# First units with gate products in pairs and a short warm-up, and MLP pieces through four stages, in a fused attention, MLP and expert kernel

## The chip, the cores and the metric

The kernel runs on one core of a Trainium2 chip, as one program. The metric is the device time of one execution in microseconds (us), the median of several executions. The engines are named as in the profile: PE (TensorE), PEld (its weight loads), DVE (VectorE), ACT (ScalarE), POOL (GpSimd) and SP (SyncE, which here only issues DMAs). A matmul's result stands in PSUM, eight banks of 128 partitions by 512 words; GpSimd is never given a PSUM operand here.

## The reference, cut to what matters

Three layers follow one another over 3072 tokens (4 sequences of 768) with 384 features (8 heads of 48):

```
# 1. linear attention with decay, per batch and head
y[t] = r[t] @ (state + (u * k[t]) outer v[t])
state = w[t][:, None] * state + k[t] outer v[t]
# 2. MLP:            x = (relu(x @ w_in) ** 2) @ w_out          384 -> 2048 -> 384
# 3. experts, top 1 of 8, on tokens with x @ w_skip > 0
out = x + prob * (relu(x @ w1[e]) @ w2[e])                      384 -> 1024 -> 384
```

All inputs and outputs are float32. The kernel takes each large product as three: every operand is split into a rounded high half (ScalarE's copy) and the low half that is left (a subtraction), and hi x hi, hi x lo and lo x hi are summed (`three`, line 565).

## The kernel before, in words

**Chunks and units.** The 768 time steps are cut into 6 chunks of 128 steps. A unit is one chunk of one sequence, four units a chunk, 24 in all. `chunk(i, par, c, cg)` is written out on every engine: its loop over f = 0 to 15 computes the MLP of chunk i, one block of 128 hidden features a turn (`layer1` on TensorE, `relu` on ScalarE, `square` on VectorE, `square_hi` and `square_lo`, and `layer2` two turns later), and between the pieces `side(n, ...)` with n = 2f and 2f+1 puts the attention of the four units of chunk c = i+1, eight steps a unit, and the routing of chunk i-1. Chunks 1 to 4 are a hardware loop; chunk 0 and the last are written out. Before chunk 0 stands a part of its own, the first four units, whose attention nothing of the MLP accompanies. It is there that most of the change lies.

**One unit.** DMAs bring r, k and the decays w with time along the free axis (`load_rk`, `load_decays`), v, and r and k once more with time along the partitions (`load_own`). VectorE takes the running product of the decays (`decays`, L1108) and its reciprocal in two halves (`inverse`, L1119). GpSimd multiplies (`factors`): r by the running product (L1472), then r by k and by u in the "own" rows (L1477, L1479), then k by the inverse (L1481). VectorE sums the own rows by head (`own_term`, L1139), and ScalarE puts those sums on the diagonal of the score tiles, eight copies (`own_diagonal`, L928). TensorE multiplies k by r (`head_scores`, L617), VectorE copies the scores under a mask over the diagonals (`mask_scores`, L1127), TensorE transposes k (`k_transpose`, L626), multiplies scores by v (`attention`, L646 to L662) and k by v (`growth`, L686). ScalarE takes k and the attention's high half out of PSUM (`take_k` L906, `take_xhi` L915), VectorE the low half and the new state (`take_xlo` L1169, `grow_state` L1153). An engine works through its own list in order; semaphores are the only thing that orders engines among themselves.

**Order before chunk 0.** TensorE begins with `keep_busy(8)`: matmuls whose results nobody reads, 8 of 512 columns (L773) and 32 of 128 columns (L777), the second kind on tiles that GpSimd clears. Then, unit by unit: scores, three gate products, from unit 2 on a gate turn, transposes, attention, growth. VectorE does decays and inverses of units 0 and 1 before unit 0's mask, and then in each unit those of the unit two later.

**The gate.** The router's weights are carried through the MLP: w_out times w_gate (with w_skip as further columns) is computed once and appended to w_out. w_out comes transposed in four pieces (n = 0 to 3) through `x2[0]` and `x2[1]`. `gate_product(n, k)` (L697) is one of three matmuls of a piece, 512 columns each, into ACC[0]; ScalarE copies the sum out (`take_gate`, L1008, after `own_diagonal` of the next unit), the next piece's first product waits for that copy, and `gate_turn(n)` (L706) turns it by four transposes. `wo_hi` and `wo_lo` then take the result (L1019, L1353), which `layer2(0, 0)` waits for.

**The MLP's weights.** Eight pieces of 768 KB, w_in and w_out by turns, k = 0 to 7. Each goes through a stage, `stage[k % 2]`: SP loads it when GpSimd has taken the low half of piece k-2 (`load_mlp_piece`, L386), ScalarE copies the high half (`split_hi`, L894), GpSimd subtracts, in three or four parts (`split_lo`, L1499), and counts `w_lo`. Pieces 0 and 1 are split before chunk 0, the high halves of 2 to 7 in chunk 0 at f = 1, 2, 4, 6, 8 and 10. Layer 1 waits for `w_lo` 1, 3, 5, 7 at f = 0, 4, 8, 12 and layer 2 for 2, 4, 6, 8. One queue, SP's, issues all these loads in a written order; an issue that waits holds every one behind it.

## Time and profile before

| | us |
|---|---|
| median of 3 runs | 813.08 (812.76 to 816.14) |
| the profiled execution's own time | 818.62 |
| its span | 817.0 |
| TensorE busy in the span | 775.0 (95%), 5539 matmuls |
| VectorE, ScalarE, GpSimd busy | 455.4, 325.3, 279.8 |
| mean granted clock of TensorE | 0.978 |
| time from span start to the MLP's first matmul | 55.78 |

The busy shares are over the whole span, in which the stages have different limits. The part before the MLP's first matmul is 7% of the span; its limits are seen only in the timelines of the engines. The granted clock is a share of TensorE's full speed: 1.00 is the upper of its two levels, 2.4 GHz, and 0.50 the lower, 1.2 GHz. The starts of instructions are those of the profile; where a line stands for several instructions, its length runs from the first one's start to the last one's end.

### The profile page before, as it was taken

How to read it: one execution, taken by the hardware profiler on the slowest of the kernel's cores; microseconds unless marked ns; L12 is line 12 of the kernel's file. 1: busy time of each engine (PE TensorE's matmuls, PEld its weight loads, DVE VectorE, ACT ScalarE, POOL GpSimd, SP SyncE). 2: the span in 40 equal slices, each digit the busy share in tenths (PEclk: the TensorE clock that was granted, in tenths of full speed). 3: DMA queues.
4: the chain of work that ended last, by engine and by line, in shares of the span. 5: the costliest groups of instructions: out<-in, count | busy, mean ns of one | idle time of the engine just before them, and what ended most of it. 6: DMA issues, size and time to landing. Idle time of an engine off the chain costs nothing.

```text
span 817.0 us, 15673 instructions
## 1 busy us (share of the span) xinstructions
PE 775.0 (95%) x5539; PEld 668.8 (82%) x5539; DVE 455.4 (56%) x733; ACT 325.3 (40%) x629; POOL 279.8 (34%) x280
## 2 busy tenths in 40 slices
PE   7879999999999998999999999999899999999884
PEld 4357788888888887888888898998799999999774
DVE  7757876766676665766586635334422244244841
ACT  1444443433343333433343324343422255255621
POOL 6366662222224220522142310282420025241840
PEclk9889999999999999999999999999899999999988
DMA  8762522422233223322232005344432136445610
GB/s 260 221 185 60 151 63 59 128 59 59 60 97 89 60 59 102 89 59 59 82 105 52 16 25 193 134 148 166 156 126 68 58 126 204 149 136 175 244 36 7
DMA packets 52351, 88.31 MB, mean 108 GB/s; under 512 B 5948, under 2 KB 33832, under 8 KB 52272
## 3 DMA queue, kind: packets, MB, share of 16 engines
q1 hardware_dynamic: 42192, 62.19, 26.6%
q0 software_dynamic: 5504, 16.44, 5.6%
q10 hardware_dynamic: 4576, 8.65, 3.1%
q8 instruction: 46, 0.75, 0.4%
q14 instruction: 33, 0.27, 0.1%
HBM read 72.98 MB, written 16.75 MB: 110 GB/s over the span
## 4 chain that ended last, share of the span: by engine, by line
PE 90%; issue 4%; DVE 3%; ACT 3%; DVEq 0%; POOL 0%; POOLq 0%; ACTq 0%
PE bank L567 26%; PE bank L569 24%; PE bank L568 24%; PE bank L617 3%; PE bank L825 2%; PE bank L662 2%; PE bank L646 2%; PE bank L697 1%; ACT spare L928 1%; PE bank L686 1%; PE bank L626 1%; PE bank L773 1%; PE bank L764 1%; PE bank L651 1%; PE bank L656 1%
## 5 line engine op out<-in xcount | busy, mean ns | idle before, releaser
L567 PE MATMUL bank<-wo_hi,h_hi 128*128 128x394 f32 (+1 forms) x576 | 202.1, 351 | 1.6 <-DVE h_lo L1396 1.5
L569 PE MATMUL bank<-wo_hi,h_lo 128*128 128x394 f32 (+1 forms) x576 | 196.6, 341 | 0.0
L568 PE MATMUL bank<-wo_lo,h_hi 128*128 128x394 f32 (+1 forms) x576 | 196.4, 341 | 0.0
L1282 DVE SCALAR_TENSOR_TENSOR hid<-bank,hid 128x512 f32<-128x512 f32 x96 | 65.1, 678 | 152.0 <-ACT hid L958 152.0
L958 ACT ACTIVATE hid<-bank 128x512 f32<-128x512 f32 x96 | 57.0, 594 | 168.3 <-PE bank L569 161.3
L567 PE MATMUL bank<-xt_hi,wi_hi 128*128 128x512 f32 x288 | 118.7, 412 | 2.2 <-issue 2.2
L1472 POOL TENSOR_TENSOR work<-work 112x512 f32<-112x512 f32 x24 | 28.4, 1185 | 257.5 <-DVE work L1108 248.3
L567 PEld LDWEIGHTS bank<-wo_hi,h_hi 128*128 128x128 f32 x576 | 109.1, 189 | 7.6 <-DVE h_lo L1396 2.2
L569 PE MATMUL bank<-xt_hi,wi_lo 128*128 128x512 f32 x288 | 113.5, 394 | 0.0
L568 PE MATMUL bank<-xt_lo,wi_hi 128*128 128x512 f32 x288 | 113.4, 394 | 0.0
L568 PEld LDWEIGHTS bank<-wo_lo,h_hi 128*128 128x128 f32 x576 | 109.1, 189 | 3.0
L569 PEld LDWEIGHTS bank<-wo_hi,h_lo 128*128 128x128 f32 x576 | 108.9, 189 | 0.0
L967 ACT ACTIVATE h_hi<-hid 128x512 fp32r<-128x512 f32 x96 | 60.6, 631 | 85.6 <-DVE hid L1282 83.8
L1119 DVE RECIPROCAL odds<-work 112x256 f32<-112x256 f32 x48 | 83.2, 1741 | 0.7
L1589 POOL DMA_INDIRECT out<-odds,y_idx x26 | 26.1, 1003 | 153.5 <-issue 142.5
L1288 DVE TENSOR_TENSOR h_lo<-hid,h_hi 128x512 fp32r<-128x512 f32 x96 | 70.5, 734 | 12.5 <-ACT h_hi L967 12.1
L928 ACT ACTIVATE spare<-ident,own_sum 128x128 f32<-128x128 f32 x192 | 58.8, 389 | 38.3 <-DVE own_sum L1139 35.6
L1232 DVE TENSOR_TENSOR xt_lo<-bank,xt_hi 128x384 fp32r<-128x384 f32 x25 | 13.9, 556 | 107.8 <-ACT xt_hi L976 107.8
L567 PE MATMUL bank<-wi_hi,xt_hi 128*128 128x512 f32 x144 | 60.3, 419 | 9.5 <-DVE xt_lo L1232 5.5
L1030 ACT ACTIVATE hid<-bank 128x512 f32<-128x512 f32 x48 | 28.7, 598 | 101.5 <-PE bank L569 98.4
L567 PEld LDWEIGHTS bank<-xt_hi,wi_hi 128*128 128x128 f32 x288 | 54.4, 189 | 16.5 <-issue 6.5
L569 PEld LDWEIGHTS bank<-xt_hi,wi_lo 128*128 128x128 f32 x288 | 54.5, 189 | 12.4
(143 smaller groups left out, 1264.7 us busy)
## 6 DMA issues: line engine op xcount, KB each, us to landing
work<-rkw SPq DMA_DIRECT2D x48, 192.0 KB, 3.6
spare<-rk_rows SPq DMA_DIRECT2D x23, 384.0 KB, 4.3
work<-v_rows SPq DMA_DIRECT2D x25, 192.0 KB, 3.9
work<-sorted_rows SPq DMA_DIRECT2D x24, 193.0 KB
work<-rkw SPq DMA_DIRECT2D x48, 96.0 KB, 3.2
x_cur<-sorted_rows SPq DMA_DIRECT2D x24, 192.0 KB
x<-w POOLq DMA_DIRECT2D x6, 768.0 KB, 6.3
work<-w ACTq DMA_DIRECT2D x6, 768.0 KB, 7.4
```

The source lines that it names most:

```text
L567: pe.matmul(ps, a_hi, b_hi, start=start, stop=False, skip_group_check=True)
L568: pe.matmul(ps, a_hi, b_lo, start=False, stop=False, skip_group_check=True)
L569: return pe.matmul(ps, a_lo, b_hi, start=False, stop=stop, skip_group_check=True)
L928: last = act.activation(scores[:, h % 2, h // 2, :], ident[:, :], ACT.Copy, scale=own_sum[:, b % 2, h:h + 1])
L958: act.activation(hid[:, f % 2, :], HID[f % 2][:, :], ACT.Relu).then_inc(sb_relu, 1)
L967: act.activation(h_hi[:, f % 3, :], hid[:, f % 2, :], ACT.Copy).then_inc(sb_hhi, 1)
L1030: act.activation(hid[:, half, :], banks[2 + half][:, :], ACT.Relu).then_inc(e_relu, 1)
L1119: dve.reciprocal(inv[0:PK, :].rearrange("p (j t) -> p j t", j=PAIRS)[:, two], by_time(cum[b % 2])[0:PK, two, 1:T + 1]).then_inc(inv_done, 1)
L1282: dve.scalar_tensor_tensor(hid[:, f % 2, :], HID[f % 2][:, :], 0.0, hid[:, f % 2, :], ALU.max, ALU.mult).then_inc(sb_sq, 1)
L1288: dve.tensor_tensor(h_lo[:, f % 3, :], hid[:, f % 2, :], h_hi[:, f % 3, :].bitcast(F32), ALU.subtract).then_inc(sb_hlo, 1)
L1472: pool.tensor_tensor(r, r, by_time(cum[n])[0:PK, :, 0:T], ALU.mult).then_inc(r_done, 1)
L1589: pool.indirect_dma_start(out=out, out_offset=bass.IndirectOffsetOnAxis(ap=y_idx[:, n:n + 1], axis=0), in_=y_out[:, n, :], in_offset=None, ...
```

## The change

- **Warm-up.** `keep_busy(3)` in place of 8, and the small matmuls go, with GpSimd's clearing of their tiles. VectorE's clearing of `state` goes to GpSimd, and VectorE waits for it before the first `grow_state`. `const_v` counts one step more, so that the loads into unit 0's tiles can start as soon as their own padding is set.
- **First loads.** Own rows of unit 0 and `u_rows` are issued before r and k. `factors(..., own_first=True)` multiplies the own rows before r in units 0 to 4.
- **VectorE's order.** Unit 0's masks come before the inverses of unit 1; in the last units scan and half of the inverse of unit (1,0) come before `take_xlo(0, 0, 3)`.
- **Gate products.** Two at a time: after unit 0's growth, then before `k_transpose` and after the gate turn of units 1 to 3, into the banks HID[0] and HID[1] by turns. ScalarE's `take_gate` comes ahead of the unit's `take_k`, and `own_diagonal` after `split_hi`. `layer1(0, f)` with f < 2 waits for the copies out of HID.
- **MLP pieces.** Four stages, `stage[0]`, `stage[1]`, `x2[0]`, `x2[1]`: piece k waits for `w_lo` of k-4, pieces 2 and 3 for the gate products that read `x2`. Their places on SP's queue and those of `split_lo` on GpSimd's list change. `take_sums(0)` waits until all pieces are split.
- **Chunk 0.** Its side steps run two places later (`late=2`): none in f = 0, and the last two after the loop.

The diff, cut to its core:

```diff
@@ semaphores and stages
-        w_loaded = [sem(f"w_loaded{n}") for n in range(2)]
+        w_loaded = [sem(f"w_loaded{n}") for n in range(4)]
+        MLP_STAGES = stage[0:2] + [x.rearrange("p b d -> p (b d)")[:, 0:STAGE] for x in x2]
...
-            return (first_piece, second_piece)[k % 2](k % 2, k // 2)
+            return (first_piece, second_piece)[k % 2](k % 4, k // 2)
@@ SP
-                if k >= 2:
-                    sp.wait_ge(w_lo, k - 1)
+                if k >= 4:
+                    sp.wait_ge(w_lo, k - 3)
+                elif k >= 2:
+                    sp.wait_ge(ps_wg, k + 1)
...
             load_decays(0, 0, 1)
-            load_rk(0, 0, 1)
+            load_own(0, 0)
             sp.wait_ge(const_v, 1)
             load_decays(0, 0, 0)
+            sp.dma_start(own_u[:, :], u_rows).then_inc(u_loaded, 16)
+            load_rk(0, 0, 1)
+            sp.wait_ge(const_v, 2)
             load_rk(0, 0, 0)
-            load_own(0, 0)
-            sp.dma_start(own_u[:, :], u_rows).then_inc(u_loaded, 16)
...
             load_transposed(1)
-            load_mlp_piece(0)
             early_decays(3)
             early_rk(2)
+            load_mlp_piece(0)
             load_mlp_piece(1)
...
             load_own(1, 0)
+            load_mlp_piece(2)
             early_v(4)
+            load_mlp_piece(3)
             early_decays(5)
             early_rk(5)
+            load_mlp_piece(4)
+            early_v(5)
+            load_mlp_piece(5)
             load_own(1, 1)
-            early_v(5)
-            load_mlp_piece(2)
-            load_mlp_piece(3)
-            load_mlp_piece(4)
+            load_mlp_piece(6)
             refill(1, 2)
-            load_mlp_piece(5)
-            load_mlp_piece(6)
             load_mlp_piece(7)
@@ PE
+                if isinstance(i, int) and i == 0 and f < 2:
+                    pe.wait_ge(sb_wg, f + 3)
...
-                    if n > 0:
-                        pe.wait_ge(sb_wg, n)
-                last = pe.matmul(ACC[0][0:NG, :], gate_w[:, k, :], transposed_piece(n)[:, k, :],
+                    if n >= 2:
+                        pe.wait_ge(sb_wg, n - 1)
+                last = pe.matmul(HID[n % 2][0:NG, :], gate_w[:, k, :], transposed_piece(n)[:, k, :],
...
+            def gate_products(first):
+                for n in range(first, first + 2):
+                    gate_product(n // KD, n % KD)
...
-            keep_busy(8)
+            keep_busy(3)
             for b in range(B):
                 head_scores(0, b)
-                if b == 0:
-                    pe.wait_ge(const_dma, 16)
-                for k in range(KD):
-                    gate_product(b, k)
-                if b > 1:
-                    gate_turn(b - 2)
+                if b > 0:
+                    gate_products(4 * b - 2)
                 k_transpose(0, b)
                 attention(0, b)
                 growth(0, b)
-            gate_turn(B - 2)
+                if b > 0:
+                    gate_turn(b - 1)
+                if b == 0:
+                    pe.wait_ge(const_dma, 16)
+                if b < B - 1:
+                    gate_products(4 * b)
             gate_turn(B - 1)
-            chunk(0, 0, 1, None)
+            chunk(0, 0, 1, None, 2)
@@ ACT
             for b in range(B):
+                if b > 0:
+                    take_gate(b - 1)
                 take_k(0, b)
                 take_xhi(0, 0, b)
-                own_diagonal((b + 1) // B, (b + 1) % B)
-                take_gate(b)
+                if b == B - 1:
+                    take_gate(b)
+                    act.wait_ge(ps_wg_turned, 4)
+                    act.activation(wo_hi[:, :, DM:], WG_PS, ACT.Copy).then_inc(wg_hi, 1)
                 if b in (1, 2):
                     split_hi(b - 1)
+                own_diagonal((b + 1) // B, (b + 1) % B)
@@ DVE
-            dve.memset(state[:, :, :, :], 0.0)
...
+            decays(0, 0)
+            inverses(0, 0)
+            own_term(0, 0)
+            decays(0, 1)
             mask_scores(0, 0, 0)
             mask_scores(0, 0, 1)
+            inverses(0, 1)
             own_term(0, 1)
+            dve.wait_ge(state_cleared, 1)
+            for b in range(2):
                 take_xlo(0, 0, b)
                 grow_state(0, b)
+                decays(0, b + 2)
+                mask_scores(0, b + 1, 0)
+                mask_scores(0, b + 1, 1)
+                inverses(0, b + 2)
+                own_term(0, b + 2)
+            take_xlo(0, 0, 2)
+            grow_state(0, 2)
+            mask_scores(0, 3, 0)
+            mask_scores(0, 3, 1)
+            decays(1, 0)
+            inverse(1, 0, 0)
+            take_xlo(0, 0, 3)
+            grow_state(0, 3)
+            own_term(1, 0)
+            inverse(1, 0, 1)
@@ POOL
-            pool.memset(h_lo[:, 0, 0:T].bitcast(F32), 0.0)
-            pool.memset(h_hi[:, :, :].bitcast(F32), 0.0).then_inc(h_clear, 1)
+            pool.memset(state[:, :, :, :], 0.0).then_inc(state_cleared, 1)
...
-            for b in range(B):
-                factors(0, b)
+            for b in range(3):
+                factors(0, b, own_first=True)
             split_lo(0)
-            factors(1, 0)
+            factors(0, 3, own_first=True)
             split_lo(1)
+            factors(1, 0, own_first=True)
+            split_lo(2)
             factors(1, 1)
-            for k in (2, 3, 4):
+            for k in (3, 4):
                 split_lo(k)
```

## Rows read from the trace of the kernel before

**Rows 1.** The page: the chain that ended last, by engine.

```profile
PE 775.0 (95%) x5539; PEld 668.8 (82%) x5539; DVE 455.4 (56%) x733; ACT 325.3 (40%) x629; POOL 279.8 (34%) x280
PEclk9889999999999999999999999999899999999988
PE 90%; issue 4%; DVE 3%; ACT 3%; DVEq 0%; POOL 0%; POOLq 0%; ACTq 0%
```

**Rows 2.** Chain that ended last, 0 to 110 us: start us, length us, what.

```profile
5.29 9.57 PE bank L773 x16
...
55.78 0.73 PE bank L567
```

**Rows 3.** TensorE in order of time: start, length, operation, idle time before.

```profile
18.31 1.16 PE L617 MATMUL bank<-work 48*128 48x128 f32 x16
...
27.21 4.43 PE L697 MATMUL bank<-x,gate_w 128*10 128x512 f32 x6 [1.91 <-ACT hid L1008]
...
46.55 2.73 PE L697 MATMUL bank<-x,gate_w 128*10 128x512 f32 x6 [1.91 <-ACT hid L1008]
...
55.19 0.60 PE L706 MATMUL bank<-ident,hid 10*128 10x10 f32 x4 [3.16 <-ACT hid L1008]
...
59.85 1.91 PE L617 MATMUL bank<-work 48*128 48x128 f32 x16
...
75.33 0.40 PE L567 MATMUL bank<-xt_hi,wi_hi 128*128 128x512 f32 x1
...
78.93 1.16 PE L617 MATMUL bank<-work 48*128 48x128 f32 x16 [1.35 <-issue]
```

**Rows 4.** VectorE in order of time, same columns.

```profile
5.26 1.23 DVE L1108 TENSOR_TENSOR_SCAN work<-work,odds 112x516 f32<-112x516 f32 x1
...
11.48 1.81 DVE L1108 TENSOR_TENSOR_SCAN work<-work,odds 112x516 f32<-112x516 f32 x1
...
19.64 1.33 DVE L1127 COPY_PREDICATED spare<-before,bank 128x512 f32<-128x512 int32 x2 [2.94 <-PE bank L617]
...
28.12 3.35 DVE L1119 RECIPROCAL odds<-work 112x256 f32<-112x256 f32 x2
...
40.91 0.49 DVE L1139 TENSOR_REDUCE own_sum<-spare 128x8 f32<-128x384 f32 x1
...
43.63 0.56 DVE L1169 TENSOR_TENSOR xt_lo<-bank,xt_hi 128x384 fp32r<-128x384 f32 x1 [2.23 <-ACT xt_hi L915]
44.11 0.71 DVE L1153 TENSOR_TENSOR spare<-bank,work 48x192 f32<-48x192 f32 x2
...
47.16 1.36 DVE L1127 COPY_PREDICATED spare<-before,bank 128x512 f32<-128x512 int32 x2
```

**Rows 5.** GpSimd in order of time, same columns.

```profile
4.45 1.37 POOL L1534 MEMSET h_hi<- 128x1536 f32 x1
...
8.91 0.99 POOL L1477 TENSOR_TENSOR spare<-spare 128x384 f32<-128x384 f32 x1 [1.09 <-DMA odds<-u_rows]
...
10.94 1.26 POOL L1481 TENSOR_TENSOR work<-work,odds 112x512 f32<-112x512 f32 x1
...
70.68 4.24 POOL L1499 TENSOR_TENSOR wi_lo<-stage,wi_hi 128x512 fp32r<-128x512 f32 x3
```

**Rows 6.** ScalarE in order of time, same columns.

```profile
24.16 2.43 ACT L928 ACTIVATE spare<-ident,own_sum 128x128 f32<-128x128 f32 x8
...
33.27 0.49 ACT L915 ACTIVATE xt_hi<-bank 128x384 fp32r<-128x384 f32 x1 [0.51 <-PE bank L656]
...
146.60 0.25 ACT L985 ACTIVATE logits<-bank 128x10 f32<-128x10 f32 x2 [0.70 <-PE bank L569]
```

**Rows 7.** Stretches of 2 us: PE, PEld, DVE, ACT, POOL busy, clock, DMA.

```profile
28.00:30.00 2.00, 2.00 (x4) 0.38 (x3) 2.00 (x3) 0.00 (x0) 1.92 (x3) 0.50 1.05 385
...
56.00:58.00 2.00, 2.00 (x5) 1.54 (x5) 0.32 (x1) 0.13 (x1) 0.66 (x1) 0.50 0.84 300
```

**Rows 8.** DMA issues over the span: what, KB each, median us to landing.

```profile
x<-w_out_t SPq DMA_DIRECT2D x4, 768.0 KB, 7.1
```

More of the change, by code:

```diff
@@ L746, in side, with chunk @@
                     rows_transpose(0)
-            def chunk(i, par, c, cg):
+            def chunk(i, par, c, cg, late=0):
                 for f in range(NF):
                     layer1(i, par, f)
-                    side(2 * f, c, cg)
+                    side(2 * f - late, c, cg)
                     if f >= 2:
@@ L754, in chunk @@
                     if f < NF - 1:
-                        side(2 * f + 1, c, cg)
+                        side(2 * f + 1 - late, c, cg)
                 layer2(i, NF - 2)
-                side(2 * NF - 1, c, cg)
+                for n in range(2 * NF - 1 - late, 2 * NF):
+                    side(n, c, cg)
                 layer2(i, NF - 1)
@@ L773, in keep_busy @@
                     pe.matmul(HID[1][:, :], before[:, :], start_col[:, 0:512], start=True, stop=True)
-                pe.wait_ge(h_clear, 1)
-                for q in range(4 * n):
-                    cols = slice(q % 4 * T, q % 4 * T + T)
-                    pe.matmul(HID[1][:, 0:T], h_hi[:, q % 3, cols], h_lo[:, 0, 0:T], start=True, stop=True)
-            keep_busy(8)
+            keep_busy(3)
             for b in range(B):
                 head_scores(0, b)
-                if b == 0:
-                    pe.wait_ge(const_dma, 16)
-                for k in range(KD):
-                    gate_product(b, k)
-                if b > 1:
-                    gate_turn(b - 2)
+                if b > 0:
+                    gate_products(4 * b - 2)
                 k_transpose(0, b)
@@ L980, in take_sums @@
                 act.wait_ge(ps_acc, NF * i + NF)
+                if isinstance(i, int) and i == 0:
+                    act.wait_ge(w_lo, MLP_PIECES)
                 if not (isinstance(i, int) and i < 2):
@@ L987, in take_sums, with chunk @@
                     act.activation(x2[par][:, b, 0:DM], ACC[b][:, 0:DM], ACT.Copy).then_inc(x2_act, 1)
-            def chunk(i, par, c, cg, c_last=False):
+            def chunk(i, par, c, cg, c_last=False, late=0):
                 for f in range(NF):
@@ L997, in chunk @@
                     relu(i, f)
-                    side(2 * f, c, cg, par, c_last)
+                    side(2 * f - late, c, cg, par, c_last)
                     square_hi(i, f)
-                    side(2 * f + 1, c, cg, par, c_last)
+                    side(2 * f + 1 - late, c, cg, par, c_last)
+                for n in range(2 * NF - late, 2 * NF):
+                    side(n, c, cg, par, c_last)
                 take_sums(i, par)
@@ L1296, in take_sums @@
             def take_sums(i, par):
+                if isinstance(i, int) and i == 0:
+                    dve.wait_ge(w_lo, MLP_PIECES)
                 if not (isinstance(i, int) and i < 2):
@@ L1301, in take_sums, with chunk @@
                     dve.tensor_copy(x2[par][:, b, 0:DM], ACC[b][:, 0:DM]).then_inc(x2_dve, 1)
-            def chunk(i, par, c, cg, c_last=False):
+            def chunk(i, par, c, cg, c_last=False, late=0):
                 for f in range(NF):
                     square(i, f)
-                    side(2 * f, c, cg, par, c_last)
+                    side(2 * f - late, c, cg, par, c_last)
                     square_lo(i, f)
-                    side(2 * f + 1, c, cg, par, c_last)
+                    side(2 * f + 1 - late, c, cg, par, c_last)
+                for n in range(2 * NF - late, 2 * NF):
+                    side(n, c, cg, par, c_last)
                 take_logits(i)
@@ L1354, in _ @@
                               ).then_inc(wg_lo, 1)
-            chunk(0, 0, 1, None)
+            chunk(0, 0, 1, None, late=2)
             dve.memset(x_cur[:, :], 0.0).then_inc(ahead_blank, 1)
@@ L1463, in wait_alone, with factors @@
                 pool.sem_inc(waits_held, 1)
-            def factors(c, b):
+            def factors(c, b, own_first=False):
                 unit = B * c + b
@@ L1469, in factors, with receptance @@
                 r, k = (rk_in[n][0:PK, a] for a in range(2))
-                pool.wait_ge(loaded[n], (2 * c + b // 2) * 32 + 32)
-                pool.wait_ge(cum_done, unit + 1)
-                pool.tensor_tensor(r, r, by_time(cum[n])[0:PK, :, 0:T], ALU.mult).then_inc(r_done, 1)
+                first = isinstance(c, int) and unit == 0
+                def receptance():
+                    pool.wait_ge(loaded[n], (2 * c + b // 2) * 32 + 32)
+                    pool.wait_ge(cum_done, unit + 1)
+                    pool.tensor_tensor(r, r, by_time(cum[n])[0:PK, :, 0:T], ALU.mult).then_inc(r_done, 1)
+                if not own_first:
+                    receptance()
                 pool.wait_ge(own_loaded[n], (2 * c + b // 2) * 16 + 16)
-                if isinstance(c, int) and unit == 0:
+                if first:
                     pool.wait_ge(u_loaded, 16)
@@ L1542, in _ @@
             pool.sem_inc(x_loaded, 32)
-            for b in range(B):
-                factors(0, b)
+            for b in range(3):
+                factors(0, b, own_first=True)
             split_lo(0)
-            factors(1, 0)
+            factors(0, 3, own_first=True)
             split_lo(1)
+            factors(1, 0, own_first=True)
+            split_lo(2)
             factors(1, 1)
-            for k in (2, 3, 4):
+            for k in (3, 4):
                 split_lo(k)
```

46 lines of the change are left out of this document (19 added, 27 removed).

## The prediction

> **What bounds the kernel now.** I read the page first: TensorE carries 90% of the chain that ended last, so only its pauses, its slow stretches and work nobody needs are to be won [rows 1]. Then the chain in order of time: from 5.29 us it is the warm-up, 9.57 us of wide matmuls and then small ones until the scores at 18.3, and the MLP's first matmul starts only at 55.78 [rows 2, 3]. That is where the change works, so I read the engines up to there one by one [rows 3 to 6].
>
> Three things show. First, the warm-up holds TensorE until 18.3, while unit 0's last input, GpSimd's product with the inverses, is ready at 10.94+1.26 = 12.20 [rows 3, 5]. Second, from unit to unit TensorE pauses 1.91 us before its gate products, since ScalarE copies the last ones out behind own_diagonal (2.43 us); after the pause the products may take 4.43 us instead of 2.73, with the granted clock at 0.50, the lower level, 1.2 GHz [rows 3, 6, 7]. The masks on VectorE end at 19.64+1.33 = 20.97 for unit 0 and 47.16+1.36 = 48.52 for unit 3 [rows 4], so 9.2 us a unit. Third, TensorE pauses another 3.16 us before the last gate_turn [rows 3], and the first layer-1 stretch runs at 0.50 [rows 7]. Chunk 0's last sums are there at 146.6: it takes 90.8 us [rows 2, 6].
>
> **Up to the first mask.** Three of eight warm-up matmuls are 3/8 x 9.57 = 3.6 us, and the second kind (14.86 to 18.3) goes. VectorE no longer clears the state, so the warm-up starts some 1.3 us sooner and ends near 7.6: off the path. GpSimd clears the state (1536 columns, as its 1.37 us clear of h_hi, which goes [rows 5]): no change there. Late next is the product with the inverses. GpSimd's first product waited to 8.91 for u_rows [rows 5]; u's issue moves ahead of both rk loads and of a wait, about 1.8 us, so I take 7.1. Two own products at 0.99 and two wide ones at 1.26 give 11.6. Bounds: u no earlier (13.4), or the own rows landing late, 1 us more. TensorE has paused nearly 4 us by then, longer than the 3.16 that went before the slow stretch, so I price the scores at 1.9 (the row at 59.85), not 1.16 (the row at 18.31) [rows 3]: 13.4. Mask 1.33: it ends at 14.8 instead of 20.97, **6.2 earlier**.
>
> **Unit to unit.** The inverses of unit 1 no longer stand ahead of mask 0 on VectorE but behind it. Each period is then VectorE's own work: inverses 3.35, own_term 0.49, x_lo 0.56, state 0.71, scan 1.23, mask 1.36 [rows 4], 7.7 us and about 0.6 of gaps. Beside the inverses and own_term (3.85) TensorE and ScalarE turn the mask into x_hi: from the end of the gate products at 27.21+4.43 = 31.64 to the copy's end at 33.76 it was 2.1 us [rows 3, 6], 3.2 at the lower clock; covered. Two gate products stand between scores and k_transpose: 4 of 6 instructions, 1.8 us of 2.73 or 2.95 of 4.43. The mask (1.36) hides most; the rest, 0.4 to 1.6, eats VectorE's cover of 1.7 (0.6 at the lower clock), so it costs 0 to 1.0 a unit; I take 0. ScalarE's gate copy now comes ahead of take_k and uses HID, so nothing waits for own_diagonal; its split_hi(0), moved ahead of own_diagonal(0,2), ends before own_term's sum is there. First period 8.3, so mask 1 ends at 23.1.
>
> Second period: split_lo(0) now lies ahead of factors(0,3), so it runs beside scan (0,3). The trace has a scan of 1.81 instead of 1.23 that began during GpSimd's product and could end only after it [rows 4, 5]. The Trainium skill, "SBUF — State Buffer", Who interferes with whom, has a VectorE instruction with two SBUF inputs blocked for the whole of a GpSimd instruction that reads SBUF; this scan agrees (12.20+1.23 = 13.4 against its end at 13.3). By a proportional sharing the cost would be some tenths; by that rule it is up to one part of the split. A split of three parts takes 4.24 [rows 5], 1.4 a part; I take 0.4, range 0 to 1.4. Mask 2 ends at 31.8.
>
> Third period: inverses to 35.2, k product 36.5, scores 37.6; own_term 35.7, own_diagonal (2.43) 38.2; mask to **39.6**. A second condition: w_out_t's last piece is issued after unit 1's state (near 28.5) and takes 7.1 to land [rows 8]: 35.6, its product ends by 36.5, just before the scores. It has no slack; 3 us later would be 3 us lost. So mask 3 ends 48.52-39.6 = 8.9 earlier, 2.7 of it here.
>
> **To the first layer 1.** It was 55.78-48.52 = 7.3 us: transposes and attention, own_diagonal(1,0), gate copy, last turn. Now the copy comes ahead of own_diagonal and layer 1 waits for neither the turn nor it. TensorE and ScalarE need to 41.8. VectorE does the scan of unit (1,0), beside split_lo(1) (1.8 by the row above), and one reciprocal (1.7) first, 43.1, then x_lo: **43.6**. 4.0 us, 3.2 fewer. Chunk 0 starts 12.2 earlier.
>
> **Inside chunk 0.** I carried the order through to layer 1 of f = 4. Before, that began at 75.33, 19.55 after the start, some 2.7 of it the lower clock (half of the 4.1 us to the scores at 59.85, and their 1.9 for 1.16) [rows 2, 3]. Now own_term and own_diagonal(1,0) come between: VectorE to 44.6, ScalarE 47.0, relu 0 at 47.6, split_hi(2) (1.5), relu 1 at 50.9, mask (1,0) at 53.0. TensorE without side work in f = 0 is at k_transpose by 50.8 and waits 2.1. If the clock falls in the 1.8 us before the start (of the pauses of 1.91 one was followed by 4.43, one by 2.73), the wait swallows the loss. Layer 1 of f = 4 then starts near 62.5, 19.0 after the start: 0.5 won. From there I keep the old rest, 71.2: it still holds the pause of 1.35 [rows 3] and six splits on GpSimd beside VectorE. Bounds -2 (no collision) to +2 (worse ones).
>
> Pieces: w_lo 3 comes when split_lo(2) ends. It needs w_hi 3 at 50.3, so 54.6, 8 us before its use. Pieces 3 and 2 load into x2 once the last gate products have read it (35 to 39.5) and land by 46. Each later split is asked for two f or more after ScalarE's copy of the same piece, which keeps its place in the chunk, so they move with it. take_sums' new wait for w_lo 8 asks for what layer 2 of f = 12 has already had. All nothing; a price only if the first fails (below).
>
> At the end two late side steps put own_diagonal (2.43) between ScalarE's last square and take_sums: relu of chunk 1 comes 3.4+0.6 after the last sums instead of 2.15+0.6, of which 0.6 had been slack: **0.7 lost**. Later chunks are unchanged.
>
> **Sum.** 12.2+0.5-0.7 = 12.0. The profiled execution had a span of 817.0 and took 818.6; that gives 806.6, against its own. The median of the runs is 813.1, 5.5 below the profiled one; I take the same 12.0 off it: 801.1.
>
> **Rivals.** (A) *Products and clock eat the pauses.* With short bursts TensorE stays at 1.2 GHz, products cost 2.95 and each of three units loses 1.0 (3.0), and the w_out_t piece lands 2.5 late: 5.5. For: no cover in the third period. Against: the new pauses are mostly about 1.5 us, and the one of 1.35 at 78.93 was followed by scores at 1.16 [rows 3]. 12-5.5 = 6.5 won, 806.6.
> The Trainium skill, "TensorE: Matmul & The Clock Gate", What's actually happening, says that the clock is granted only to sustained activity; here 28 to 30 us stand at 0.50 after a pause of 1.91 [rows 3, 7], which agrees and speaks for A.
> (B) *Collisions vanish.* VectorE's stops beside the splits fall elsewhere, the pause of 1.35 and the 2.1 wait shrink: 4 more, 797.
> (C) *The weights hold chunk 0.* If the third piece's low half stays where it was, 70.68+4.24 = 74.92 [rows 5], layer 1 of f = 4 starts at 74.9 and nearly all is given back: 812.7.
> (D) *Slower*: the same place, but piece 2, waiting on SP's queue behind unit 3's own rows and a gate product, lands so late that w_lo 3 passes 75.3. Each us beyond is lost; with 3 us, 816. Against: it would have to be 20 us later than I find.
>
> **Chances.** Forecast (797.5 to 804) 0.60, A 0.20, B 0.12, C 0.05, D 0.03. Range 796 to 808 leaves B's low and C and D out. The measurement tells 0.5%, 4.1 us, from no change: slower 0.03; same 0.05, from C and A's upper end; faster 0.92.
>
> **What would show it.** Scores of unit 0 near 11.6; masks ending near 14.8, 23, 32 and 40; first layer 1 near 43.6; layer 1 of f = 4 near 62.5; last sums of chunk 0 near 134. Masks 10 us apart would show A; w_lo 3's split ending after 62 would show C. I am wrong if VectorE is not what the units wait for.

## The result, and the profile after

The changed kernel takes 803.84 us (median of 4 runs, 802.69 to 806.81), the kernel before 814.54 us beside it (4 runs). The ratio is 0.9875, 95% interval 0.9837 to 0.9913: 10.2 us less, with 7 to 13 us in the interval. A later comparison of the same two kernels gave 0.9915 (0.9885 to 0.9946), 7 us less. Forecast were 801.1 and 12.0 less.

The two profiled spans differ by more, 817.0 to 802.1 us. But 6.0 us of these 14.9 lie behind the last chunk, where nothing was changed: from chunk 5's last sums to the end it was 259.0 and 253.0 us in these two profiles, and 253 to 261 in the others of this study, whichever kernel ran. So single profiles are compared below up to the sums of chunk 1, the first point at which all that the change touches is over.

The page of the changed kernel first, its busy line and its chain [rows 1]; nothing in them tells the two kernels apart, since both are 95% TensorE:

```profile
PE 764.3 (95%) x5497; PEld 660.7 (82%) x5497; DVE 453.1 (56%) x732; ACT 324.6 (40%) x629; POOL 285.1 (36%) x279
...
PE 89%; DVE 4%; issue 3%; ACT 2%; DMA 1%; POOL 0%; DVEq 0%; SPq 0%; POOLq 0%; ACTq 0%
```

VectorE before chunk 0 (start, length, operation, idle time before) [rows 4]:

```profile
6.59 1.23 DVE L1129 TENSOR_TENSOR_SCAN work<-work,odds 112x516 f32<-112x516 f32 x1 [2.70 <-DMA work<-rkw]
...
14.87 1.34 DVE L1148 COPY_PREDICATED spare<-before,bank 128x512 f32<-128x512 int32 x2 [1.22 <-PE bank L624]
...
24.31 1.36 DVE L1148 COPY_PREDICATED spare<-before,bank 128x512 f32<-128x512 int32 x2 [1.47 <-PE bank L624]
...
30.54 4.50 DVE L1129 TENSOR_TENSOR_SCAN work<-work,odds 112x516 f32<-112x516 f32 x1
35.06 1.34 DVE L1148 COPY_PREDICATED spare<-before,bank 128x512 f32<-128x512 int32 x2
...
42.68 1.36 DVE L1148 COPY_PREDICATED spare<-before,bank 128x512 f32<-128x512 int32 x2 [1.53 <-ACT spare L940]
43.92 1.78 DVE L1129 TENSOR_TENSOR_SCAN work<-work,odds 112x516 f32<-112x516 f32 x1
```

The masks end at 16.2, 25.7, 36.4 and 44.0, where I had 14.8, 23.1, 31.8 and 39.6. The scan of unit 3 stands out: 4.50 us for 1.23. GpSimd and TensorE beside it [rows 5, 3]:

```profile
7.75 1.00 POOL L1516 TENSOR_TENSOR spare<-spare 128x384 f32<-128x384 f32 x1 [2.06 <-DMA odds<-u_rows]
...
11.30 1.27 POOL L1522 TENSOR_TENSOR work<-work,odds 112x512 f32<-112x512 f32 x1 [0.35 <-DVE odds L1140]
...
30.22 3.72 POOL L1540 TENSOR_TENSOR wi_lo<-stage,wi_hi 128x512 fp32r<-128x512 f32 x3
34.73 1.09 POOL L1516 TENSOR_TENSOR spare<-spare 128x384 f32<-128x384 f32 x1 [0.79 <-DMA spare<-rk_rows]
```

```profile
12.62 2.08 PE L624 MATMUL bank<-work 48*128 48x128 f32 x16 [3.37 <-POOL work L1522]
...
19.88 3.17 PE L704 MATMUL bank<-x,gate_w 128*10 128x512 f32 x4
...
32.45 1.89 PE L704 MATMUL bank<-x,gate_w 128*10 128x512 f32 x4 [0.97 <-DMA x<-w_out_t]
...
48.01 0.47 PE L572 MATMUL bank<-xt_hi,wi_hi 128*128 128x512 f32 x1 [0.79 <-issue]
```

Unit 0's scores take 2.08 us and the first two gate products 3.17, both at the lower clock; the fourth pair, products 6 and 7, which are the first to read w_out_t's third piece, waits 0.97 us for it; unit 3's own rows arrive at 34.7; the MLP starts at 48.01 instead of 55.78, 7.7 us earlier (forecast 12.2). Then the ends of chunks 0 and 1 on ScalarE [rows 6]:

```profile
138.16 0.22 ACT L1001 ACTIVATE logits<-bank 128x10 f32<-128x10 f32 x2
...
221.68 0.25 ACT L1001 ACTIVATE logits<-bank 128x10 f32<-128x10 f32 x2 [0.77 <-PE bank L574]
```

and of the kernel before:

```profile
231.85 0.25 ACT L985 ACTIVATE logits<-bank 128x10 f32<-128x10 f32 x2 [0.77 <-PE bank L569]
```

Chunk 1's sums come at 221.68; in the kernel before it was 231.85, so 10.2 us are won there. TensorE's first matmul of chunk 1, changed and before:

```profile
135.83 0.39 PE L572 MATMUL bank<-xt_hi,wi_hi 128*128 128x512 f32 x1
```

```profile
146.41 0.40 PE L567 MATMUL bank<-xt_hi,wi_hi 128*128 128x512 f32 x1
```

TensorE goes on to chunk 1 at 135.8 and not, as before, at 146.4; the sums stand at 138.2 because own_diagonal now lies ahead of them. By TensorE, chunk 0 is 87.8 us long instead of 90.7.

The DMA engines are what I had not looked at. Stretches of the changed kernel, then of the kernel before (busy time of PE, PEld, DVE, ACT, POOL, granted clock, mean busy share of the DMA engines, GB/s):

```profile
14.00:20.00 6.00, 4.43 (x61) 3.24 (x58) 5.13 (x6) 1.25 (x4) 3.05 (x4) 0.50 1.10 318
20.00:36.00 16.00, 13.23 (x104) 5.06 (x102) 14.21 (x15) 8.17 (x21) 10.89 (x10) 0.92 1.03 302
```

```profile
20.00:36.00 16.00, 12.88 (x147) 6.24 (x145) 10.87 (x16) 7.11 (x22) 4.41 (x4) 0.89 0.70 215
```

From 14 to 36 us the mean share is 1.03 to 1.10, which is full; before, it was 0.70 in the second stretch. The shorter start asks for as many bytes in less time: 12.4 MB in the 48 us before chunk 0, where it was 12.2 MB in 56 us.

### The profile page after: what moved, and what is told of

The parts are those of the page before. It is cut to its first block, busy times and chain, and to the rows that moved or that the text cites. A ratio compares the mean times of both kernels' runs of the same rounds, so it can differ in the third digit from the quotient of the medians.

```text
span 802.1 us, 15589 instructions
## 1 busy us (share of the span) xinstructions
PE 764.3 (95%) x5497; PEld 660.7 (82%) x5497; DVE 453.1 (56%) x732; ACT 324.6 (40%) x629; POOL 285.1 (36%) x279
## 4 chain that ended last, share of the span: by engine, by line
PE 89%; DVE 4%; issue 3%; ACT 2%; DMA 1%; POOL 0%; DVEq 0%; SPq 0%; POOLq 0%; ACTq 0%
PE bank L572 26%; PE bank L574 25%; PE bank L573 25%; PE bank L624 3%; PE bank L837 2%; PE bank L669 2%; PE bank L653 2%; PE bank L693 1%; DVE odds L1140 1%; PE bank L633 1%; PE bank L779 1%; ACT spare L940 1%; DVE spare L1148 1%; PE bank L658 1%; PE bank L663 1%
## 5 line engine op out<-in xcount | busy, mean ns | idle before, releaser
L1051 ACT ACTIVATE hid<-bank 128x512 f32<-128x512 f32 x48 | 28.7, 598 | 95.8 <-PE bank L574 95.6
L574 PEld LDWEIGHTS bank<-xt_hi,wi_lo 128*128 128x128 f32 x288 | 54.5, 189 | 12.4
```

The costliest lines, as they stand in the source:

```text
L574: return pe.matmul(ps, a_lo, b_hi, start=False, stop=stop, skip_group_check=True)
L1051: act.activation(hid[:, half, :], banks[2 + half][:, :], ACT.Relu).then_inc(e_relu, 1)
```

## The experiments

Each is told with the places that tell (us in its one profile) and with its ratio to the kernel before. Places of single profiles are to be read with care: changed, e10 and e3 are the same kernel up to the start of chunk 0, and mask 2 ends at 36.4, 32.6 and 32.1 in them. The kernel before has only one profile: in ten of the thirteen comparisons the gain read at chunk 1's sums is 1.2 to 3.8 us larger than the timed one.

| | masks 0 to 3 end | chunk 0 starts | sums of chunk 1 | ratio (95%) |
|---|---|---|---|---|
| before | 21.0, 28.2, 37.8, 48.5 | 55.7 | 231.9 | |
| changed | 16.2, 25.7, 36.4, 44.0 | 48.0 | 221.7 | 0.9875 (0.9837 to 0.9913) |
| changed, again (e10) | 14.5, 22.9, 32.6, 45.3 | 49.5 | 223.6 | 0.9915 (0.9885 to 0.9946) |
| e1 warm-up of six | 15.0, 23.0, 33.7, 43.5 | 47.7 | 221.4 | 0.9887 (0.9855 to 0.992) |
| e2 split in a pause | 16.4, 24.4, 36.5, 45.0 | 49.2 | 223.0 | 0.9913 (0.9883 to 0.9944) |
| e3 no late steps | 15.0, 23.2, 32.1, 43.5 | 47.7 | 222.5 | 0.9883 (0.9833 to 0.9933) |
| e4 before, warm-up of three | 17.1, 26.7, 34.6, 42.9 | 51.5 | 226.6 | 0.9976 (0.9945 to 1.0007) |
| e5 pieces 0, 1 later | 15.4, 24.9, 32.5, 44.9 | 49.0 | 223.7 | 0.992 (0.9894 to 0.9947) |
| e6 the same, warm-up of six | 14.6, 22.7, 30.4, 43.0 | 47.4 | 222.4 | 0.9876 (0.9834 to 0.9918) |
| e7 two stages | 15.3, 24.8, 35.6, 44.3 | 48.5 | 226.7 | 0.9969 (0.9938 to 1.0) |
| e8 before, pause filled | 21.5, 28.7, 38.3, 46.6 | 55.5 | 229.0 | 0.9982 (0.9945 to 1.0018) |
| e9 diagonals first | 14.6, 22.6, 30.3, 38.0 | 45.2 | 221.5 | 0.9908 (0.9879 to 0.9937) |
| e11 thin pieces | 14.8, 23.9, 35.5, 44.8 | 48.4 | 222.1 | 0.9922 (0.9882 to 0.9961) |
| e12 thin, warm-up of six | 14.9, 22.9, 33.6, 41.2 | 46.1 | 219.9 | 0.99 (0.9865 to 0.9935) |

**e4_before_warm3: the warm-up alone.**

```diff
-            keep_busy(8)          # 8 wide, 32 small
+            keep_busy(3)          # 3 wide, none small
```

> The kernel before with only the warm-up cut: three wide matmuls, no small ones. Theory 1 (the warm-up held unit 0, and every unit after it stands in a row): scores of unit 0 start at 12.3 instead of 18.3, but the first gate products wait for w_out_t (landing near 16) and run at the lower clock; mask 0 ends near 15.5, and chunk 0 starts 4 to 6 us earlier than 55.8. Theory 2 (later units are held by loads or by ScalarE, so the early start is lost): chunk 0 starts within 1 us of 55.8.

Chunk 0 starts 4.2 us earlier and chunk 1's sums come 5.3 us earlier: theory 1. The first gate products now wait for w_out_t, as expected. By the two profiles that is half of what the whole change brings up to that point. The timing does not bear the size out: 0.9976 is 2 us, and its interval reaches from 4.5 us won to 0.6 lost. So it is not shown that the warm-up is half of the change: the kernel before has one profile, of an execution of 818.6 us, 4 above its median.

**e1_warm6: is the warm-up too short?**

```diff
-            keep_busy(3)
+            keep_busy(6)
```

> The changed kernel with six wide warm-up matmuls in place of three, so that TensorE is busy until about 11.2 us and pauses only 1.4 us before unit 0's scores (12.6). Theory 1 (the short warm-up lets the clock fall, and this delays units 0 and 1): scores of unit 0 take 1.1 us instead of 2.1, the first two gate products 1.8 to 1.9 instead of 3.1, granted clock 1.00 from 12 to 22 us, mask of unit 1 ends 2 to 3 us earlier than 25.7, chunk 0 starts 1.5 to 3 us earlier than 48.0. Theory 2 (the gate products, whatever the clock, and VectorE's own work set it): masks within 0.7 us of where they are, no measurable difference in time.

Both were half right. Unit 0's scores take 1.16 instead of 2.08 us, the first gate products 1.88 instead of 3.17, and mask 1 ends 2.7 us earlier than in the first profile of the changed kernel. But chunk 0 starts only 0.3 earlier: on the way the fourth pair of gate products waits for w_out_t.

```profile
19.59 1.16 PE L624 MATMUL bank<-work 48*128 48x128 f32 x16 [0.64 <-POOL work L1522]
...
31.65 3.58 PE L704 MATMUL bank<-x,gate_w 128*10 128x512 f32 x4 [2.89 <-DMA x<-w_out_t]
```

How much the lower clock cost units 0 and 1 is less sure than it looks. With three warm-up matmuls, e10 and e3 have scores of 1.66 and 1.75 us and first gate products of 2.10 and 2.01, and end mask 1 at 22.9 and 23.2, where it is 22.95 here; e3 starts chunk 0 at 47.7, as this run does. So six matmuls bring 0 to 2.7 us at mask 1, by how the clock and the first loads fell, and nothing that shows at chunk 0.

**e2_split_in_pause: the scan against the split.** ScalarE copies piece 0 ahead of the first gate copy, GpSimd subtracts it between two products of unit 2.

```diff
-            for b in range(3):
-                factors(0, b, own_first=True)
-            split_lo(0)
+            for b in range(3):
+                factors(0, b, own_first=True, split=(0 if b == 2 else None))
```

> The changed kernel with the split of MLP piece 0 put into GpSimd's pause between the product with the decays and the product with the inverses of unit 2 (its high half copied by ScalarE ahead of the first gate copy), where VectorE runs its reciprocals. Theory 1 (the scan of unit 3 took 4.50 us because GpSimd's split held VectorE's second read of SBUF): the scan takes 1.2 to 1.8 us, mask 2 ends 2.5 to 3.3 us before 36.4, and chunk 0 starts 2 to 3 us before 48.0. Theory 2 (the scan waited for the decays' load or for a semaphore): it still ends near 35.0 and chunk 0 starts at 48.0 within 0.7 us.

The scan takes 2.26 us instead of 4.50: theory 1 in kind, though not the 1.2 to 1.8 expected, since the split came so late that its third part still ran when the scan began. Piece 0 itself landed late: ScalarE waited 3.11 us for it and GpSimd 2.16 us for ScalarE's copy, so unit 2's product with the inverses came at 33.0 instead of 30.3. Mask 2 stands where it was and chunk 0 starts at 49.2: the edit failed, and it was a load again.

```profile
27.19 3.72 POOL L1544 TENSOR_TENSOR wi_lo<-stage,wi_hi 128x512 fp32r<-128x512 f32 x3 [2.16 <-ACT wi_hi L906]
30.87 2.18 POOL L1526 TENSOR_TENSOR work<-work,odds 112x512 f32<-112x512 f32 x1
```

```profile
29.74 2.26 DVE L1131 TENSOR_TENSOR_SCAN work<-work,odds 112x516 f32<-112x516 f32 x1
```

Here the scan had its turn as soon as the third part ended, ahead of the product behind it, and it was the product that took 2.18 us for 1.27.

**e10_changed_again: the changed kernel once more.**

> The changed kernel once more, unedited, timed beside the run above on one chip. It should stand 9 to 11 us under the kernel before. Whether the scan of unit 3 is held (4.5 us, as in three of the profiles with this order) or not (1.2 us, as in one) tells if this collision is a matter of how the loads happen to land; either way chunk 0 should start between 47.4 and 48.5, since the own rows of unit 3 and w_out_t's third piece come at the same time.

Here the scan was not held (1.23 us: it began before the split), mask 2 ended at 32.6, 3.8 us earlier than in the first profile, and yet mask 3 ended 1.2 later. TensorE and then ScalarE and VectorE stood behind this:

```profile
27.55 1.16 PE L624 MATMUL bank<-work 48*128 48x128 f32 x16
33.30 3.58 PE L704 MATMUL bank<-x,gate_w 128*10 128x512 f32 x4 [4.58 <-DMA x<-w_out_t]
...
40.26 1.88 PE L704 MATMUL bank<-x,gate_w 128*10 128x512 f32 x4
```

w_out_t's third piece held TensorE for 4.58 us, against 0.97 in the first profile. It landed 10.9 us after its issue, against 7.3. The two holds stand in for each other. (Chunk 0 started at 49.5, a microsecond outside my 47.4 to 48.5, and the ratio gives 7 us, under my 9 to 11.)

**e5_pieces_later: the pieces not needed yet behind those that are.** Pieces 0 and 1 are issued behind the last piece of w_out_t; ScalarE copies them one unit later, and GpSimd subtracts the first after unit 3's products and the second after those of unit (1,0).

```diff
-            load_mlp_piece(0)
-            load_mlp_piece(1)
             early_v(2)
             load_transposed(2)
...
             load_transposed(3)
+            load_mlp_piece(0)
+            load_mlp_piece(1)
```

> The changed kernel with MLP pieces 0 and 1 issued behind the last piece of w_out_t in place of ahead of its third, their copies and splits one unit later on ScalarE and GpSimd. Theory 1 (units 2 and 3 are held by loads: the DMA engines are full from 3 to 36 us, and the third w_out_t piece and unit 3's own rows stand behind 1.5 MB of weights that are not needed yet): gate products 6 and 7 wait for no DMA, the scan of unit 3 is not held by a split, masks 2 and 3 end near 32 and 40, chunk 0 starts 3 to 4.5 us before 48.0. Theory 2 (VectorE's and ScalarE's own order sets unit 3): chunk 0 starts within 1 us of 48.0. Risk under either: copies and splits of the two pieces come so late that the first layer 1 or layer 2 waits for w_lo.

No wait for the third piece, scan 1.23, mask 2 at 32.5: so far theory 1. Then the risk came in, elsewhere than I had put it. ScalarE and VectorE:

```profile
39.62 1.48 ACT L906 ACTIVATE wi_hi<-stage 128x1536 fp32r<-128x1536 f32 x1 [4.86 <-DMA stage<-w_in]
41.01 2.43 ACT L940 ACTIVATE spare<-ident,own_sum 128x128 f32<-128x128 f32 x8
```

```profile
43.58 1.34 DVE L1148 COPY_PREDICATED spare<-before,bank 128x512 f32<-128x512 int32 x2 [6.32 <-ACT spare L940]
```

ScalarE waits 4.86 us for piece 0, with unit 3's diagonals queued behind it, and VectorE waits 6.32 for those. Chunk 0 starts at 49.0; the expected 3 to 4.5 us did not come.

**e6_pieces_later_warm6** is e5 with `keep_busy(6)`.

> The same with six wide warm-up matmuls instead of three. Theory 1 (once the loads are out of the way, what unit 0 and 1 gain by the upper clock is kept to the end): masks 1, 2 and 3 end 1.5 to 2.7 us earlier than in the run with three, chunk 0 starts near 42. Theory 2 (as with the loads in the old order, the gain is lost on the way): chunk 0 starts within 0.7 us of the run with three.

Masks 1 and 2 end 2.2 us earlier than in e5 and chunk 0 starts 1.6 us earlier, at 47.4: theory 1 in kind, but "near 42" missed, for ScalarE waited as in e5 (5.14 us).

**e9_diagonal_first** is e6 with that order mended.

```diff
-                if b >= 2:
-                    split_hi(b - 2)
+                if b == B - 1:
+                    split_hi(1)
                 own_diagonal((b + 1) // B, (b + 1) % B)
+                if b == 2:
+                    split_hi(0)
```

> The last version but one (pieces 0 and 1 later, six warm-up matmuls) with unit 3's diagonals ahead of the copy of piece 0 on ScalarE, and the copy of piece 1 ahead of the diagonals of unit (1,0). There VectorE waited 6.59 us for the diagonals and ScalarE, ahead of them, 5.14 us for piece 0's load. Theory 1 (only this wait still held unit 3): mask 3 ends near 38 instead of 43.0, chunk 0 starts at 42.5 to 44, and the kernel is 3 to 5 us faster than with 47.4. Theory 2 (the weights now bound: piece 0's low half is ready only at about 43, piece 1's at 53, and the own rows of unit (1,0) land at 45): chunk 0 starts near 43 but loses 2 us or more again before layer 1 of f = 4, which then comes no earlier than 64, and the kernel gains under 2 us.

Mask 3 ends at 38.0, as theory 1 said. Then VectorE waits for the decays of unit (1,0), and inside chunk 0 h_lo is held beside the splits:

```profile
36.67 1.36 DVE L1150 COPY_PREDICATED spare<-before,bank 128x512 f32<-128x512 int32 x2 [1.69 <-PE bank L624]
41.07 1.79 DVE L1131 TENSOR_TENSOR_SCAN work<-work,odds 112x516 f32<-112x516 f32 x1 [3.04 <-DMA work<-rkw]
...
55.13 2.50 DVE L1313 TENSOR_TENSOR h_lo<-hid,h_hi 128x512 fp32r<-128x512 f32 x1
...
64.60 4.00 DVE L1313 TENSOR_TENSOR h_lo<-hid,h_hi 128x512 fp32r<-128x512 f32 x1 [0.24 <-ACT h_hi L981]
```

Chunk 0 starts at 45.2, 2.9 us before the changed kernel's, and nearly all of it is lost again behind: chunk 1's sums at 221.5, against 221.7. The amount is theory 2's, but most of the loss has another cause than the weights. The long h_lo of 4.00 us stands in the changed kernel too (3.92). Layer 1 begins 2.1 us ahead of the changed kernel's at f = 4 and at f = 5 (64.58 for 66.66, 68.93 for 71.01) and 0.05 behind it at f = 6 (77.55 for 77.50). Between f = 5 and f = 6 TensorE paused 1.50 us where the changed kernel paused 0.91, and its clock fell: twelve products of layer 2 took 3.8 us for 2.3. This run, then the changed kernel:

```profile
74.00:76.00 2.00, 2.00 (x8) 2.00 (x8) 0.00 (x0) 2.00 (x7) 0.00 (x0) 0.52 1.00 216
76.00:78.00 2.00, 2.00 (x8) 1.93 (x7) 1.87 (x4) 1.24 (x3) 0.00 (x0) 0.63 1.03 217
```

```profile
74.00:76.00 2.00, 1.86 (x20) 1.77 (x21) 1.20 (x3) 1.34 (x5) 0.00 (x0) 1.00 0.37 92
76.00:78.00 2.00, 2.00 (x13) 1.91 (x12) 0.37 (x1) 1.60 (x5) 0.00 (x0) 1.00 1.02 209
```

The other 0.8 us go before f = 4, where this run stands at 0.50 from 45 to 50 us. Whether the clock falls there in every execution of this version one profile cannot say. Timed it is 0.9908, the changed kernel beside it 0.9915. No version here is faster than the changed kernel by more than the intervals.

**e11_thin_pieces and e12_thin_pieces_warm6: fewer bytes.**

```diff
+                if k < 2:
+                    raw, src = raw[:, 0:1], src[:, 0:1]
                 sp.dma_start(raw, src).then_inc(w_loaded[k % 4], 16)
...
+            dve.memset(stage[0][:, 512:STAGE], 0.0)
+            dve.memset(stage[1][:, 2 * DM:STAGE], 0.0)
```

e12 has `keep_busy(6)` besides. Both leave most of the weights of pieces 0 and 1 out of the MLP's sums.

> The changed kernel in which MLP pieces 0 and 1 load a third and a quarter of their bytes (512 and 384 of 1536 columns, the rest of each stage stays zero; the MLP's sums leave those weights out), every instruction on the five engines otherwise the same but two memsets on VectorE while it has nothing to do. 1.1 MB fewer pass the DMA engines before 28 us. Theory 1 (bytes in flight set units 2 and 3): the third w_out_t piece lands 3 us or more sooner, gate products 6 and 7 wait less than 0.5 us, unit 3's own rows are there by 32 us, and chunk 0 starts 2 to 4 us before the 48.0 and 49.5 of the two profiles of the changed kernel. Theory 2 (order and dependencies, not bytes): start of chunk 0 within those two. The split of piece 0 may hold the scan of unit 3 in either.

> The same with six wide warm-up matmuls. In the full kernel six instead of three brought mask 1 2.7 us forward and the start of chunk 0 only 0.3. Theory 1 (the loads took it back): here 1.5 us or more of it reach chunk 0, which starts near 42 to 44. Theory 2 (something else takes it back): again within 0.7 us of the thin version with three.

In e11 the third piece of w_out_t is there in time and unit 3's own rows wait for nothing, as theory 1 said, but chunk 0 starts at 48.4. In place of the loads stands the collision, the longest of all:

```profile
28.73 5.43 DVE L1131 TENSOR_TENSOR_SCAN work<-work,odds 112x516 f32<-112x516 f32 x1
```

```profile
28.41 3.71 POOL L1544 TENSOR_TENSOR wi_lo<-stage,wi_hi 128x512 fp32r<-128x512 f32 x3
32.08 1.00 POOL L1520 TENSOR_TENSOR spare<-spare 128x384 f32<-128x384 f32 x1
```

With six warm-up matmuls (e12) the start of chunk 0 is 2.3 us earlier than in e11, where the full kernel's was 0.3: theory 1 by its number, though the start is 46.1 and not 42 to 44. But mask 1 is only 1.0 us earlier (22.9 for 23.9), so no more than that can be the warm-up's; the rest came between the masks, where the scan took 4.48 for 5.43 us and the third piece again held TensorE, for 1.57. Chunk 1's sums, at 219.9, are the earliest of all runs; timed, it is not ahead of the others (0.99). Bytes are one of the two holds, and neither alone sets the end.

**e7_two_stages: the four stages undone.** Two stages and SyncE's old order for the pieces from the second on.

```diff
-            return (first_piece, second_piece)[k % 2](k % 4, k // 2)
+            return (first_piece, second_piece)[k % 2](k % 2, k // 2)
...
             load_own(1, 0)
-            load_mlp_piece(2)
             early_v(4)
-            load_mlp_piece(3)
             early_decays(5)
             early_rk(5)
-            load_mlp_piece(4)
+            load_own(1, 1)
             early_v(5)
-            load_mlp_piece(5)
-            load_own(1, 1)
-            load_mlp_piece(6)
+            load_mlp_piece(2)
+            load_mlp_piece(3)
+            load_mlp_piece(4)
             refill(1, 2)
+            load_mlp_piece(5)
+            load_mlp_piece(6)
             load_mlp_piece(7)
```

With two stages every piece from the second on waits again for the low half of the piece two before it.

> The changed kernel with the MLP pieces through two stages again and their loads in the old places of SyncE's queue; all else stays. Theory 1 (chunk 0 now starts too early for two stages: pieces 2 and 3 are issued at about 49.5 and land at 55 to 59, behind ScalarE's need at 53.4 and 56.6, so relu 1 and 2 are held): start of chunk 0 as in the changed kernel, layer 1 of f = 4 2 to 4 us later than 66.7, the sums of chunk 0 2 to 4 us later than 138.2. Theory 2 (four stages are worth nothing, the weights always had room): all within 0.7 us.

Chunk 0 starts at 48.5 and chunk 1's sums come at 226.7, 178.2 us after it; in the changed kernel it is 173.7 and 174.1. So the stages and the order are worth 4 to 4.5 us, once the chunk starts this early: theory 1, a little more than its 2 to 4. The timing agrees (0.9969, where the changed kernel has 0.9875 and 0.9915). ScalarE shows where the first of it goes; another 1.9 us go from layer 1 of f = 9 to that of f = 10, which takes 7.4 us for 5.5:

```profile
53.51 0.63 ACT L979 ACTIVATE h_hi<-hid 128x512 fp32r<-128x512 f32 x1 [0.76 <-DVE hid L1303]
56.48 1.49 ACT L904 ACTIVATE wi_hi<-stage 128x1536 fp32r<-128x1536 f32 x1 [2.34 <-DMA stage<-w_in]
```

**e3_late0: the late side steps undone.**

```diff
-            chunk(0, 0, 1, None, 2)
+            chunk(0, 0, 1, None, 0)      # on TensorE, ScalarE and VectorE
```

> The changed kernel with chunk 0's side steps two places earlier again, as in the kernel before. Theory 1 (the two places are worth nothing here): TensorE waits some 2 us for the product with the inverses of unit (1,0), ready at 52.2, ahead of the scores, instead of 2.1 us for the mask; layer 1 of f = 4 starts within 0.7 us of 66.7, and the 0.5 us at the seam to chunk 1 come back: 0 to 1 us faster. Theory 2 (the shift is what shortened chunk 0 from 90.8 to 87.9): chunk 0 gets 2 to 3 us longer.

From chunk 0's start to chunk 1's sums it is 174.8 us, against 173.7 and 174.1: the two places are worth 0.7 to 1.1 us, between the theories. Layer 1 of f = 4 came at 68.2, 20.5 us after the start against 18.7 and 19.1, and not within 0.7 us of 66.7 as theory 1 had it; some of this is the clock, 0.50 from 54 to 56 us here after a pause of 1.89 us. The timing (0.9883, 0.9833 to 0.9933) does not tell it from the changed kernel. Its part before chunk 0 is the changed kernel's, and there too w_out_t held TensorE (3.61 us) and the scan was free.

**e8_before_filler: the clock at chunk 0's start.**

```diff
             gate_turn(B - 2)
+            for _ in range(2):
+                pe.matmul(HID[1][:, :], before[:, :], start_col[:, 0:512], start=True, stop=True)
             gate_turn(B - 1)
```

> The kernel before with two idle matmuls of 512 columns put into TensorE's pause of 3.16 us before the last gate_turn. Theory 1 (the lower clock after this pause is the main thing that made chunk 0 2.9 us longer than in the changed kernel): granted clock 1.00 from 56 to 61 us, and the sums of chunk 0 come 2.2 to 2.9 us earlier than 146.6 with the start unchanged at 55.8. Theory 2 (other waits stand in its place): the sums less than 1 us earlier.

```profile
56.00:58.00 2.00, 2.00 (x12) 1.41 (x12) 0.22 (x1) 0.17 (x1) 0.00 (x0) 1.00 0.79 271
```

The clock is 1.00 where it was 0.50 [rows 7], and chunk 0's sums come at 143.7 instead of 146.6 with the start 0.3 earlier: 2.6 us, theory 1. All of it is won before layer 1 of f = 4, which begins 17.0 us after the start instead of 19.6. Chunk 1's sums come 2.9 earlier. In this profile a pause filled with useless matmuls is worth a quarter of the whole change; the timing (0.9982, 0.9945 to 1.0018) is 1.5 us and does not tell it from nothing.

## Why the prediction was right, and where its terms were not

The direction, the size and most of the mechanism came out: 10.2 us (7 in the repetition) for 12.0. By the steps:

- *Up to the first mask*, 6.2 forecast: 4.8 and 6.4 in the two profiles. The scores went to the lower clock as priced (1.9 forecast, 2.1 and 1.7 measured). u_rows landed for 7.75 (6.56 in the second), not 7.1; in the first profile the second half of the decays came late (scan at 6.59 for 5.3).
- *Unit to unit*, 2.7 more: the first profile kept 4.5 for mask 3 and the second 3.2, where 8.9 had been forecast. So instead of a gain of 2.7 from mask 0 to mask 3 there was a loss of 0.3 and of 3.2: this is the term that was mis-sized, by 3 and 6 us. The sentence "I take 0.4, range 0 to 1.4" gave the scan one part of the split; it waited for all three, 3.3 us, and in e11 for four GpSimd instructions.
- *The other hold, in the same term*: "It has no slack; 3 us later would be 3 us lost" saw the kind of the other hold but not its place: it spoke of w_out_t's last piece in the third period, and the piece that held was the third, in the second. It was priced at the 7.1 us median of the trace before. There the third piece took 6.1 us to land; in the changed kernel it took 7.3 and 10.9, in e1 and e3, which load in the same order, 9.9. With pieces 0 and 1 behind it (e5) it took 4.4 and with thin pieces (e11) 5.7, so those 1.5 MB are the main part of its delay, though with thin pieces and six warm-up matmuls (e12) it took 8.6. The waits were 0.97 us, then 2.9, 3.6 and 4.6 in e1, e3 and e10. I had put this into rival A, with the clock as its main cause; by e1 and e3, which both start chunk 0 at 47.7, the clock of the first units cost little up to there, and the bytes much. (Of the three pauses of 1.91 us in the trace before, two were followed by products of 4.43 us; the prediction counted one of two.)
- *To the first layer 1*: 4.0 us forecast and 4.0 measured in the first profile (44.04 to 48.01), 4.2 in the second.
- *Inside chunk 0*: 0.5 forecast, 2.9 in the first profile and 2.5 in the second (137.7 to 146.4 on TensorE, 6.2 of it from the start). Up to layer 1 of f = 4 the sum came out: 18.7 and 19.1 us after the start for 19.0 forecast and 19.6 before (the 2.7 us priced for the lower clock there are e8's 2.6). What was mis-sized is "the old rest", kept at 71: on TensorE it is 69.2 in both profiles for 71.1. It is not the late side steps, for e3 has 68.9 without them. Part of it is what rival B names: the state's second product on VectorE took 3.44 us beside a split before, and the pause behind it was 1.35 us, where the changed kernel has 2.69 and 0.91. The rest stays open. "The wait swallows the loss" was borne out by e10: its clock was 0.50 from 50 to 52 us, and chunk 0 was 88.3 us long, against 87.8 at the full clock.
- *The pieces* at nothing: in neither profile does TensorE wait for w_lo. e7 shows that they would have cost 4 to 4.5 us otherwise. That is a loss of rival C's kind and the four stages kept it away, but it arises where ScalarE copies piece 2 (2.34 us of wait), and layer 1 of f = 4 comes at 69.8 and not at C's 74.9.
- *The seam*: 0.7 lost forecast, 0.4 measured (10.6 won at TensorE's entry to chunk 1, 10.2 at chunk 1's sums).

So two terms were off in opposite directions, -4.5 (the start) and +2.4 us (chunk 0); with 0.3 at the seam that makes 10.2 of 12.0. That the total fits within 2 us is in part luck.

What stays open: the share of each hold in the timed difference. The two profiles of the changed kernel differ by 1.9 us at chunk 1's sums, and by which hold they show; no run had both taken away and nothing put in their place (e9 had the next load and two slow stretches of the clock instead).

## What to carry to other kernels

When a start-up stage is shortened, its bytes stay: look at the DMA share of that stretch first, and price a load's landing by the share it will meet, not by its median in the slower kernel. Where two waits end within a microsecond of one another, taking one away shows the other; count a gain only up to the second. And a subtraction cut into parts gave the other engine no turn between its parts: put such a chain where the other engine reads only one operand from SBUF. In e2 the split lay beside xt_lo and the state's sums, which read one operand from PSUM, and they kept their 0.56 and 0.71 us.

## What the hardware showed that I had not expected

- VectorE's scan, which has two SBUF inputs, waited through a whole chain of GpSimd instructions: 3.3 us beside a split of three parts (30.22 to 33.94), 4.2 beside the same split and the product that followed it (28.41 to 33.1). The Trainium skill, "SBUF — State Buffer", SBUF: two separate sides, says that whichever starts first has the shared pair for the whole instruction. The trace agrees that it blocks, but the instruction that waited did not get its turn when the first GpSimd instruction ended. That is no fixed order either: in e2 the scan, begun in the split's third part, went ahead of the product behind it. The loser can also be GpSimd: in e3 the scan began 0.25 us before the split, took its 1.23 us, and the split took 4.49 for 3.72.
- The clock fell again inside chunk 0 of e9 (0.52 and 0.63 from 74 to 78 us) after a pause of 1.50 us; after 0.91 us at the same place it did not in the changed kernel. Pauses of 1.91 us were followed by the lower clock twice in the kernel before (4.43 us of gate products) and once not (2.73).
- The same code met its loads at other times from run to run: 5.3 to 6.6 us for the first scan, 0.6 to 4.6 us of wait for one piece (0.57 in e7, 4.58 in e10). The stage's length changed less (47.7 to 49.5 us): the holds replaced one another.
- The expert part took 253 to 261 us in 14 profiles, whatever the kernel; a difference of two single spans says nothing at the 1% level here.
